# The local band of the first 288 tokens as dense blocks on TensorE, ahead of two MLPs

## Chip, cores and metric

One core of a Trainium2 chip runs the program. The metric is the device time of one execution in microseconds (us), the median over several runs. The engines are TensorE (PE; PEld is its weight load), VectorE (DVE), ScalarE (ACT), GpSimd (POOL) and SyncE (SP), which issues most DMAs.

## What is computed

For 4 batches, 8 heads, 576 tokens and 64 dimensions, each head adds two attentions. The coarse one works on means of four tokens (144 by 144); its result is repeated four times. The local one lets each query see the keys at a distance under four, a band of seven. The sum is a matrix of 2304 tokens by 512, which goes through two MLPs of width 2048.

```python
q_d = q.reshape(B, H, Sd, factor, D).mean(axis=3)      # k_d, v_d likewise, factor = 4
out_up = np.repeat(sm_attn(q_d, k_d, v_d), factor, axis=2)
mask = np.abs(pos[:, None] - pos[None, :]) < factor
scores = np.where(mask, scale * np.matmul(q, k.transpose(0, 1, 3, 2)), -1e9)
out = out_up + softmax(scores) @ v
r = np.maximum(x @ w_in, 0.0);  y = (s * (r * r) + b) @ w_out
h = y @ w_in2;  result = (h - np.tanh(h)) @ w_out2
```

## The kernel before

A batch is cut into two subs of 288 tokens, eight in all (s = 0 to 7). In the first MLP one sub is one tile of 288 columns (j = 0 to 7); the second MLP has six tiles of 384 columns. Every product runs as three products of split parts: a high part (`wah`, `wbh`, `xh`, `gh`) and a low part, the rest (`wal`, `wbl`, `xl`, `gl`).

**Band.** The partition holds a head pair and a chunk of 18 tokens. Sub 0 has the first nine tokens of every chunk, sub 1 the last nine, so each sub has tokens from all over the sequence. VectorE multiplies queries by seven shifted keys and sums over 64 dimensions (`key_products`, `key_sums`, in four units of 5, 5, 4 and 4 tokens), forms the softmax (`band_max`, `band_norm`, with the exponential on ScalarE) and multiplies and adds the values (`value_products`, `value_sums`). TensorE transposes the result (`columns`), and VectorE adds the coarse part `up` and writes `xraw` (`add_up`).

**Coarse attention.** POOL and VectorE add up groups of four tokens (`group_sums`), TensorE transposes them, and for each of eight steps (four head pairs, two halves of 72 queries) come `scores`, `score_max` (VectorE, tile `cneg`), `score_exp`, `score_inverse`, `score_scale`, `turn_probs` (a transpose), `place_probs`; `weigh` and `place_up` follow once per head pair.

**First MLP.** A turn is one of 16 slices f of the width: `hidden1` (12 products), then ScalarE's `activate1` (relu, `gh`, square), POOL's `g_low` (`gl`), then `output1` (12 products), three turns behind. Tile 0 needs each weight slice in two parts. ScalarE makes the high one (`w1_high`, L968). The low one is made for f under 8 (`FTURN`) by TensorE, as identity times raw minus high (`w1_rest`), and by ScalarE, which places it (`w1_place`); for the others by POOL (`w1_low`). Weights come in quarters of four slices, 1 MB each: `wa_raw` of `w_in`, `wb_raw` of `w_out`.

**Order.** Each engine runs its own list strictly in order. A planner (`Plan`) writes the lists out ahead of time from estimated costs and ranks. PE's small results go through two PSUM banks in turn (`pa`). A wait at the head of a list holds up all behind it. `add_up` of sub s waits until `hidden1` of tile s - 2 is done (`XRING`).

## Time and profile before

| | |
|---|---|
| median of 3 runs | 956.36 us (952.87 to 957.5) |
| the profiled execution | 955.23 us, its span 953.4 us |
| TensorE busy | 900.6 us, 94% |
| VectorE, ScalarE, POOL busy | 547.5, 429.6, 301.5 us |
| mean granted TensorE clock | 0.978 of full speed |

The profile is of one execution. Times count from the span's start. A row of a timeline has its start, its length, engine, line, operation, output<-input and count, and in square brackets how long the engine was idle before it and what ended that. A row by line has busy time, mean ns, and idle time before it. A row by stage reads, after the stretch and its length: busy us (and instruction count) of PE, PEld, VectorE, ScalarE and POOL, then the granted clock of TensorE as a share of 2.4 GHz, the busy share of the 16 DMA engines, and GB/s. Rows overlap on an engine by a few hundredths of a microsecond. A matmul in plain fp32 shows as two records.

### The profile page before, as it was taken

Reading aid. Unit: us, or ns where it says so; the run is one execution under the profiler, and the core shown is the slowest. Engines: PE = TensorE matmul, PEld = TensorE weight load, DVE = VectorE, ACT = ScalarE, POOL = GpSimd, SP = SyncE. Lnnn points to the kernel's source line nnn. Section 1 sums busy time; section 2 is a strip of 40 time slices with the busy share of each in tenths; the row PEclk is TensorE's granted clock in tenths of the full one; section 3 lists DMA queues with packets and bytes.
Section 4 is the critical chain, followed back from the end, with each engine's and each line's share of the span. In section 5 each row is a group of like instructions: output and inputs, shape, how many; then the busy total and the mean of one; then the engine's idle time right before and its main releaser. Section 6 shows DMA issues by size and latency. Waiting matters only on the chain.

```text
span 953.4 us, 14703 instructions
## 1 busy us (share of the span) xinstructions
PE 900.6 (94%) x5600; PEld 830.6 (87%) x5600; DVE 547.5 (57%) x630; ACT 429.6 (45%) x1081; POOL 301.5 (32%) x285
## 2 busy tenths in 40 slices
PE   1789879998999999999999999999999999999997
PEld 0348869998999899999999999999999999999996
DVE  6889999999998999983100462332332423322321
ACT  1688446455765477544645662322322323222221
POOL 6308975588747973344222200000000000000000
PEclk9779989999999999999999999999999999999999
DMA  9996024243424222201204430110100200100101
GB/s 226 260 240 145 25 72 132 59 123 99 111 61 124 62 71 67 68 1 34 92 1 148 153 103 1 34 34 1 55 12 1 67 1 1 34 1 1 34 1 33
DMA packets 35973, 66.47 MB, mean 70 GB/s; under 512 B 3920, under 2 KB 16192, under 8 KB 35904
## 3 DMA queue, kind: packets, MB, share of 16 engines
q1 hardware_dynamic: 33968, 62.39, 24.4%
q10 hardware_dynamic: 1936, 3.15, 1.5%
q8 instruction: 44, 0.72, 0.3%
q14 instruction: 25, 0.20, 0.1%
HBM read 56.09 MB, written 9.44 MB: 69 GB/s over the span
## 4 chain that ended last, share of the span: by engine, by line
PE 80%; DVE 9%; ACT 3%; issue 2%; DMA 2%; SPq 1%; POOL 1%; DVEq 0%; ACTq 0%
PE hid L1275 21%; PE acc L1293 21%; PE hid L1234 17%; PE acc L1256 17%; DVE prod L860 3%; DMA wa_raw<-in_moe_w_in_dram 2%; DVE prod L868 2%; DVE prod L873 1%; PE pa L1177 1%; PE pa L1202 1%; PE acc L1166 1%; DVE oloc L878 1%; PE pa L1188 1%; PE pa L1214 1%; SPq L618 1%
## 5 line engine op out<-in xcount | busy, mean ns | idle before, releaser
L740 POOL TENSOR_TENSOR gl<-relu,gh 128x288 fp32r<-128x288 f32 x128 | 146.3, 1144 | 193.8 <-PE acc L1256 160.0
L928 DVE TENSOR_TENSOR gdif<-hid,tanh 128x384 f32<-128x384 f32 x96 | 53.5, 557 | 184.8 <-ACT tanh L1115 184.8
L1234 PE MATMUL hid<-xh,wah 128*128 128x288 f32 x512 | 156.1, 306 | 0.0
L1256 PE MATMUL acc<-gh,wbh 128*128 128x288 f32 (+1 forms) x512 | 156.0, 305 | 0.0
L1234 PE MATMUL hid<-xh,wal 128*128 128x288 f32 x512 | 152.3, 299 | 0.0
L1256 PE MATMUL acc<-gl,wbh 128*128 128x288 f32 (+1 forms) x512 | 151.9, 297 | 0.0
L1256 PE MATMUL acc<-gh,wbl 128*128 128x288 f32 (+1 forms) x512 | 151.7, 296 | 0.0
L1234 PE MATMUL hid<-xl,wah 128*128 128x288 f32 x512 | 149.0, 298 | 1.8 <-POOL xl L731 1.8
L1115 ACT ACTIVATE tanh<-hid 128x384 f32<-128x384 f32 x96 | 47.1, 490 | 187.4 <-PE hid L1275 187.1
L1275 PE MATMUL hid<-x2h,wal 128*128 128x384 f32 x384 | 129.1, 336 | 0.0
L1275 PE MATMUL hid<-x2h,wah 128*128 128x384 f32 x384 | 129.0, 336 | 0.0
L1275 PE MATMUL hid<-x2l,wah 128*128 128x384 f32 x384 | 129.0, 336 | 0.0
L1074 ACT ACTIVATE relu<-hid 128x288 f32<-128x288 f32 x128 | 52.4, 409 | 148.5 <-PE hid L1234 141.2
L1293 PE MATMUL acc<-wbl,g2h 128*128 128x512 f32 x288 | 112.6, 391 | 0.0
L1293 PE MATMUL acc<-wbh,g2l 128*128 128x512 f32 x288 | 112.5, 391 | 0.0
L1293 PE MATMUL acc<-wbh,g2h 128*128 128x512 f32 x288 | 112.3, 390 | 0.0
L1256 PEld LDWEIGHTS acc<-gh,wbh 128*128 128x128 f32 x512 | 97.4, 190 | 2.4 <-issue 1.4
L1234 PEld LDWEIGHTS hid<-xh,wah 128*128 128x128 f32 x512 | 98.0, 191 | 1.6 <-issue 0.7
L1234 PEld LDWEIGHTS hid<-xl,wah 128*128 128x128 f32 x512 | 96.7, 191 | 2.3 <-POOL xl L731 2.3
L1234 PEld LDWEIGHTS hid<-xh,wal 128*128 128x128 f32 x512 | 98.0, 191 | 0.7
L1256 PEld LDWEIGHTS acc<-gh,wbl 128*128 128x128 f32 x512 | 97.1, 190 | 0.6
L1256 PEld LDWEIGHTS acc<-gl,wbh 128*128 128x128 f32 x512 | 96.9, 189 | 0.0
...
## 6 DMA issues: line engine op xcount, KB each, us to landing
...
ql<-in_q_dram SPq DMA_DIRECT2D x28, 144.0 KB, 3.2
```

The source lines that it names most:

```text
L618: sp.dma_start(stage_of(b, n).rearrange("p (h x) -> p h x", h=2), dram(v, b * BSTEP + 2 * hq * HSTEP + kh * HG * GROUP * HD, [[GROUP * HD, ...
L740: g.tensor_tensor(out=gl[:, turn % LRING1, 0:NS], in0=relu[:, f % 2, :], in1=gh[:, turn % GRING1, 0:NS].bitcast(F32), op=ALU.subtract).the ...
L860: ve.tensor_tensor(prod[:, 0:nt, :, :], vv, pv, ALU.mult).then_inc(s_mul, 1)
L868: ve.tensor_tensor(prod[:, 0:nt, 0:3, :], prod[:, 0:nt, 0:3, :], prod[:, 0:nt, 3:6, :], ALU.add).then_inc(s_tree, 1)
L873: ve.tensor_tensor(pairs, pairs, others, ALU.add).then_inc(s_tree, 1)
L928: ve.tensor_tensor(gdif[:, f % 2, :], hid[:, f % 2, 0:N2], tanh[:, f % 2, :], ALU.subtract).then_inc(s_dif, 1)
L1074: sc.activation(r, hid[:, f % 2, 0:n], ACT.Relu).then_inc(s_relu, 1)
L1115: sc.activation(tanh[:, f % 2, :], hid[:, f % 2, 0:N2], ACT.Tanh).then_inc(s_tanh, 1)
L1234: one = pe.matmul(dst, w[:, d, cols], x[:, j % XRING, d, :], start=i == 0, stop=i == len(products) - 1)
L1256: one = pe.matmul(acc[:, d, n], w[:, f, cols], g[:, turn % ring, n], start=(f == 0 and p == 0), stop=(f == FT - 1 and p == 2))
L1275: one = pe.matmul(hid[:, f % 2, 0:N2], w[:, d, f * P:(f + 1) * P], x[:, j % 2, d, :], start=(d == 0 and p == 0), stop=(d == KT - 1 and p = ...
L1293: one = pe.matmul(acc[:, i, :], g[:, f % GRING2, i * P:(i + 1) * P], w[:, f, :], start=(f == 0 and p == 0), stop=(f == FT - 1 and p == 2))
```

## The change

The tokens of batch 0 are split otherwise: sub 0 has tokens 0 to 287 in their own order, sub 1 the other 288, nine to a partition. Sub 0's band is no longer made on VectorE. For each head pair a (four):

- `dense_turn`: TensorE transposes keys and queries (three transposes each); VectorE copies the keys (`dense_keys`), ScalarE the queries (`dense_queries`), the two heads in separate columns.
- `dense_scores`: five products, each 60 queries of both heads by 66 keys.
- `dense_max`, `dense_exp`, `dense_norm`: mask, softmax over 66 columns, on VectorE, with the exponential on ScalarE.
- `dense_probs`, `dense_place`: five transposes, and ScalarE's copy.
- `dense_values`: ten products; `dense_add`: VectorE adds `up` and writes `xraw`. After it `xh` of this head pair may be made.

Keys, queries and values of sub 0 are loaded by token instead of by chunk, 64 floats at a time. The coarse attention of batch 0 does its first 72 queries for all four head pairs, then, behind the dense path, the other 72, with eight `weigh` steps of half the width. Tiles of the dense path lie where later weights go, so `wb_raw` of the last two quarters and `wbh` from f = 4 on wait for it. Low parts are now made by POOL in 24 of 32 cases and by TensorE in 8 (`low_maker`), and through `pa`. The add-up of sub 1 takes 15 instructions instead of 5. Stores of batch 0's rows follow the new order.

```diff
+BLOCKS, BSTEP1, BQ = 5, 57, 60
+BK = BQ + 2 * HALO
+BKEY0 = [0] + [BSTEP1 * i - HALO for i in range(1, BLOCKS)]
+DTOK = NS // 3
+DKEY = NS + HALO
...
+def low_maker(f, half):
+    return ("POOL", "POOL", "POOL", "PE")[(f + half) % 4]
...
+def score_of(b, i):
+    return (i % NPAIR, i // NPAIR) if b == 0 else (i // 2, i % 2)
+def weighs(b):
+    return 2 * NPAIR if b == 0 else NPAIR
...
+            if half and f >= WGROUP:
+                after.append(("dense_values", NPAIR - 1))
+            o.add("ACT", act(512), (2, f + 3 * half) if f + 3 * half > 3 else (1, 0, 5), ("w1_high", f, half), after)
+            maker = low_maker(f, half)
+            if maker == "PE":
+                o.add("PE", 1.1, (0, 9, f), ("w1_rest", f, half), [("w1_high", f, half)], 0.5, fills=True)
+                o.add("ACT", act(512), (0, 9, f), ("w1_low", f, half), [("w1_rest", f, half)],
+                      empties=("w1_rest", f, half))
...
+        o.add("DVE", 0.5, (0, 0, 30 + 0), ("dense_keys", a), [("dense_turn", a)] + ring)
...
+        o.add("PE", 2.4, (0, 0, 30 + 3), ("dense_values", a), [("dense_place", a), ("load_dense_values",)]
+              + {1: [("dense_keys", 3)], 2: [("dense_queries", 3)], 3: [("dense_add", 0)]}.get(a, []))
+        o.add("DVE", 0.55, (0, 0, 0), ("dense_add", a), [("dense_values", a), ("place_up", 0, a)])
...
+            if b == 0 and qh:
+                after.append(("dense_add", NPAIR - 1))
...
+    def tokens_of(s):
+        return (NS, SUB) if s == 1 else (s % NSUB * SUB, CHUNK)
...
+            elif kind == "load_dense_keys":
+                for j in range(3):
+                    sp.dma_start(dkey[0:DTOK, j, :, :], dram(k, j * HD, [[3 * HD, DTOK], [HSTEP, HEADS], [1, HD]])
+                                 ).then_inc(s_dkey, 16)
+                sp.dma_start(dkey[DTOK:DTOK + 1, :, :, :], dram(k, NS * HD, [[HD, 3], [HSTEP, HEADS], [1, HD]])
+                             ).then_inc(s_dkey, 16)
+            elif kind == "load_dense_queries":
+                for j in range(3):
+                    sp.dma_start(dqry[0:DTOK, j, :, :], dram(q, j * HD, [[3 * HD, DTOK], [HSTEP, HEADS], [1, HD]])
+                                 ).then_inc(s_dqry, 16)
...
+            elif kind == "load_dense_values":
+                for i in range(BLOCKS):
+                    sp.dma_start(dval[0:BK, i, :, :], dram(v, BKEY0[i] * HD, [[HD, BK], [HSTEP, HEADS], [1, HD]])
+                                 ).then_inc(s_dval, 16)
...
+                ve.tensor_tensor(pr[:, 0, :], s[:, 0, :], dmask[:, 0, :], ALU.add).then_inc(s_dmax, 1)
+                ve.tensor_tensor(pr[:, 1:BLOCKS, :], s[:, 1:BLOCKS, :],
+                                 over(dmask[:, 1, :], [[0, BLOCKS - 1], [1, BK]]), ALU.add).then_inc(s_dmax, 1)
+                ve.wait_ge(s_dmax, 4 * a + 2)
+                ve.tensor_reduce(mx, pr, AX_X, ALU.max).then_inc(s_dmax, 1)
+                ve.wait_ge(s_dmax, 4 * a + 3)
+                ve.tensor_tensor(pr, pr, over(mx, [[1, BLOCKS], [0, BK]]), ALU.subtract).then_inc(s_dmax, 1)
...
+                ve.tensor_reduce(sm, dprob[:, a % 2, :, :], AX_X, ALU.add).then_inc(s_dnorm, 1)
+                ve.wait_ge(s_dnorm, 3 * a + 1)
+                ve.reciprocal(iv, sm).then_inc(s_dnorm, 1)
+                ve.wait_ge(s_dnorm, 3 * a + 2)
+                ve.tensor_tensor(pr, pr, over(iv, [[1, BLOCKS], [0, BK]]), ALU.mult).then_inc(s_dnorm, 1)
...
+                ve.tensor_tensor(four(xraw[:, 0, a, :]), four(dense_out(a)),
+                                 over(up[:, a, 0:HG], [[1, HG], [0, GROUP]]), ALU.add).then_inc(s_dadd, 1)
...
+                if s == 1:
...
+                    for i, (t, c, group, chunks, groups) in enumerate(parts):
...
+                        uv = over(up[:, 0:1, group:group + 1], [[GROUPS, NPAIR]] + groups)
+                        ve.tensor_tensor(xv, pv, uv, ALU.add).then_inc(
+                            s_free[r] if i == len(parts) - 1 else s_added, 1)
...
+                sc.wait_ge(s_dmax, 4 * a + 4)
+                pr = dprob[:, a % 2, :, 0:BK]
+                sc.activation(pr, pr, ACT.Exp).then_inc(s_dexp, 1)
...
+                sc.activation(dpT[0:BK, a % 2, 0:4, :], acc[0:BK, 2, :].rearrange("p (i n) -> p i n", n=P), ACT.Copy
+                              ).then_inc(s_dpT, 1)
...
+                for j in range(3):
+                    one = pe.transpose(hid[:, 0, j * (DTOK + 1):(j + 1) * (DTOK + 1)],
+                                       pair(dkey[0:DTOK + 1, j, 2 * a:2 * a + 2, :]), ident[0:DTOK + 1, 0:DTOK + 1])
...
+                for i in range(BLOCKS):
+                    one = pe.matmul(acc[:, a % 2, i * BK:(i + 1) * BK], dqT[:, a % 2, i, :],
+                                    dkT[:, a % 2, BKEY0[i]:BKEY0[i] + BK], start=True, stop=True)
...
+                for i in range(BLOCKS):
+                    dst = acc[0:BK, 2, i * P:(i + 1) * P] if i < 4 else acc[0:BK, a % 2, 3 * P:4 * P]
+                    one = pe.transpose(dst, dprob[:, a % 2, i, 0:BK], ident[:, :])
...
+                for i in range(BLOCKS):
+                    n = BSTEP1 if i < BLOCKS - 1 else BQ
+                    for h2 in range(2):
+                        one = pe.matmul(dense_out(a)[h2 * HD:(h2 + 1) * HD, i * BSTEP1:i * BSTEP1 + n],
+                                        dval[0:BK, i, 2 * a + h2, :], dpT[0:BK, a % 2, i, h2 * HD:h2 * HD + n],
+                                        start=True, stop=True)
```

What the planner makes of it is seen in the lists. First the DMA queue of SyncE from the program's start, before the change; `own`, `first` and `firstv` are the coarse attention's tokens.

```order
L546 DMA kl<-in_k_dram 32x768
L546 DMA kl<-in_k_dram 31x192
L546 DMA kl<-in_k_dram 32x960
L546 DMA kl<-in_k_dram 32x2x960 x3
L613 DMA own<-in_q_dram 128x768 x2
L613 DMA first<-in_q_dram 128x768
L613 DMA first<-in_k_dram 128x768 x3
L618 DMA firstv<-in_v_dram 72x2x256 x8
L646 DMA wa_raw<-in_moe_w_in_dram 128x4x512
L655 DMA wb_raw<-in_moe_w_out_dram 128x4x512
L646 DMA wa_raw<-in_moe_w_in_dram 128x4x512
L655 DMA wb_raw<-in_moe_w_out_dram 128x4x512
```

And with the change:

```order
L736 DMA dkey<-in_k_dram 96x8x64 x3
L738 DMA dkey<-in_k_dram 1x24x64
L743 DMA dqry<-in_q_dram 96x8x64 x3
L723 DMA own<-in_q_dram 128x768 x2
L723 DMA first<-in_q_dram 128x768
L723 DMA first<-in_k_dram 128x768 x3
L748 DMA dval<-in_v_dram 66x8x64 x5
L728 DMA firstv<-in_v_dram 72x2x256 x8
L776 DMA wa_raw<-in_moe_w_in_dram 128x4x512
L613 DMA ql<-in_q_dram 32x2x576 x4
L621 DMA kl<-in_k_dram 32x2x960 x4
L776 DMA wa_raw<-in_moe_w_in_dram 128x4x512
L788 DMA wb_raw<-in_moe_w_out_dram 128x4x512
```

Three key loads, one small one, three query loads and five value loads of the dense path now stand ahead. Sub 1's `ql` and `kl` stand ahead of the second quarter of `w_in` and of the first of `w_out`. The window loads of sub 0 are gone (its `ql` and `vl` were on ScalarE's queue).

Second, ScalarE's list just ahead of tile 0, before the change (L968 makes high parts, L974 places low ones, L1065 makes `xh`):

```order
L968 ACTIVATE wbh<-wb_raw 128x512
L974 ACTIVATE wal<-acc 128x4x128
L968 ACTIVATE wah<-wa_raw 128x4x128
L968 ACTIVATE wbh<-wb_raw 128x512
L968 ACTIVATE wah<-wa_raw 128x4x128
L974 ACTIVATE wbl<-acc 128x512
L968 ACTIVATE wbh<-wb_raw 128x512
L974 ACTIVATE wal<-acc 128x4x128
L968 ACTIVATE wah<-wa_raw 128x4x128
L1065 ACTIVATE xh<-xraw 128x288 x4
L974 ACTIVATE wbl<-acc 128x512
```

And with the change (L1207 makes high parts, L1214 places low ones, L1320 makes `xh`):

```order
L1320 ACTIVATE xh<-xraw 128x288 x2
L1207 ACTIVATE wbh<-wb_raw 128x512
L1207 ACTIVATE wah<-wa_raw 128x4x128
L1295 ACTIVATE up<-pa 128x72
L1207 ACTIVATE wbh<-wb_raw 128x512
L1207 ACTIVATE wah<-wa_raw 128x4x128
L1207 ACTIVATE wbh<-wb_raw 128x512
L1207 ACTIVATE wah<-wa_raw 128x4x128
L1207 ACTIVATE wbh<-wb_raw 128x512
L1207 ACTIVATE wah<-wa_raw 128x4x128
L1320 ACTIVATE xh<-xraw 128x288
L1214 ACTIVATE wbl<-pa 128x512
```

All four `xh` stood together behind the eighth slice of the weights. Now three stand ahead, and the last one stands behind eight high parts, of which the first reads `wb_raw`.

Third, VectorE's list where sub 1 is worked on, before the change, key units and group sums:

```order
L799 TENSOR_REDUCE sc_72<-prod 128x35
L790 TENSOR_TENSOR prod<-ql,kl 128x2240
L799 TENSOR_REDUCE sc_72<-prod 128x35
L790 TENSOR_TENSOR prod<-ql,kl 128x1792
L799 TENSOR_REDUCE sc_72<-prod 128x28
L790 TENSOR_TENSOR prod<-ql,kl 128x1792
L810 TENSOR_TENSOR own<-own 128x6x64
L813 TENSOR_TENSOR qs<-own 128x192
L810 TENSOR_TENSOR own<-own 128x6x64
L813 TENSOR_TENSOR ks<-own 128x192
L799 TENSOR_REDUCE sc_72<-prod 128x28
```

And with the change:

```order
L997 TENSOR_REDUCE sc_72<-prod 128x35
L988 TENSOR_TENSOR prod<-ql,kl 128x2240
L948 TENSOR_TENSOR xraw<-acc,up 128x288
L997 TENSOR_REDUCE sc_72<-prod 128x35
L988 TENSOR_TENSOR prod<-ql,kl 128x1792
L966 TENSOR_REDUCE cneg<-pa 72x2 x2
L997 TENSOR_REDUCE sc_72<-prod 128x28
L988 TENSOR_TENSOR prod<-ql,kl 128x1792
L975 RECIPROCAL cinv<-csum 72x2 x2
L966 TENSOR_REDUCE cneg<-pa 72x2 x2
L997 TENSOR_REDUCE sc_72<-prod 128x28
L1029 SCALAR_TENSOR_TENSOR sc_72<-sc_72,mask 128x126
```

Three of the four `xraw` writes of sub 0 stand between sub 1's first key units, and the maxima of coarse steps 4 to 7 (L966) among the last ones. On TensorE the scores for the first two of these stand behind hidden turn 0, for the other two behind hidden turn 3. Further on, all six group sums of batch 1 that VectorE makes stand behind `band_norm` of sub 1; before, two stood there.

## Rows read from the trace of the kernel before

**Rows 1.** Section 1 of the page: busy time of each engine.
```profile
PE 900.6 (94%) x5600; PEld 830.6 (87%) x5600; DVE 547.5 (57%) x630; ACT 429.6 (45%) x1081; POOL 301.5 (32%) x285
```

**Rows 2.** Busy time by stage, columns as in the section on the profile.
```profile
0.00:34.90 34.90, 9.48 (x30) 4.22 (x30) 25.12 (x27) 9.52 (x32) 21.77 (x34) 1.00 0.96 234
34.90:74.00 39.10, 34.80 (x126) 18.75 (x127) 32.87 (x46) 31.83 (x90) 6.28 (x9) 0.74 1.04 246
74.00:144.00 70.00, 58.53 (x397) 54.21 (x395) 68.00 (x53) 40.22 (x108) 59.78 (x47) 0.93 0.30 75
144.00:550.70 406.70, 401.14 (x3038) 391.81 (x3037) 292.42 (x275) 231.44 (x623) 213.69 (x199) 0.99 0.30 84
550.70:953.40 402.70, 396.66 (x2016) 361.61 (x2015) 129.09 (x233) 116.62 (x230) 0.00 (x0) 1.00 0.08 22
```

**Rows 3.** Timeline of TensorE: first product of tile 0 and of tile 1.
```profile
73.95 0.29 PE L1234 MATMUL hid<-xh,wah 128*128 128x288 f32 x1
...
143.95 0.86 PE L1234 MATMUL hid<-xh,wah 128*128 128x288 f32 x1
```

**Rows 4.** VectorE by stretch: us, busy (x count), PEclk, DMA share, GB/s.
```profile
10.30:61.10 50.80, 46.54 (x54) 0.88 1.06 256
95.90:144.00 48.10, 47.52 (x37) 0.89 0.17 44
```

**Rows 5.** Chain of waits: start us, us, what.
```profile
153.95 3.19 PE hid L1234 x24
```

**Rows 6.** Timeline of VectorE, sub 1: start us, us, engine, line, operation.
```profile
89.69 2.00 DVE L799 TENSOR_REDUCE sc<-prod 128x28 f32<-128x1792 f32 x1
...
95.89 3.41 DVE L860 TENSOR_TENSOR prod<-vl,prob 128x2240 f32<-128x2240 f32 x1
99.22 1.64 DVE L810 TENSOR_TENSOR own<-own 128x384 f32<-128x384 f32 x1
100.90 0.85 DVE L813 TENSOR_TENSOR ks<-own 128x192 f32<-128x192 f32 x1
...
137.85 1.67 DVE L903 TENSOR_TENSOR xraw<-pa,up 128x256 f32<-128x256 f32 x3
```

**Rows 7.** VectorE by line, 10 to 61.2 us: busy us, mean ns.
```profile
L860 DVE TENSOR_TENSOR prod<-vl,prob 128x2240 f32<-128x2240 f32 x2 | 5.0, 2484 | 0.1
...
L878 DVE TENSOR_TENSOR oloc<-prod 128x320 f32<-128x320 f32 x2 | 1.0, 491 | 0.1
```

**Rows 8.** Timeline of ScalarE ahead of tile 0.
```profile
34.86 0.63 ACT L968 ACTIVATE wah<-wa_raw 128x512 fp32r<-128x512 f32 x1 [1.84 <-DMA wa_raw<-in_moe_w_in_dram]
...
67.39 0.62 ACT L968 ACTIVATE wbh<-wb_raw 128x512 fp32r<-128x512 f32 x1
67.91 0.62 ACT L968 ACTIVATE wah<-wa_raw 128x512 fp32r<-128x512 f32 x1
...
71.78 1.43 ACT L1065 ACTIVATE xh<-xraw 128x288 fp32r<-128x288 f32 x4
```

**Rows 9.** DMA from 35 to 40 us: packets; queue, MB, share of 16 engines.
```profile
DMA packets 944, 1.93 MB, mean 386 GB/s; under 512 B 36, under 2 KB 36, under 8 KB 944
...
q1 hardware_dynamic: 944, 1.93, 105.7%
```

**Rows 10.** DMA from 102 to 105 us, the same columns.
```profile
DMA packets 156, 0.15 MB, mean 49 GB/s; under 512 B 12, under 2 KB 156, under 8 KB 156
...
q1 hardware_dynamic: 156, 0.15, 18.5%
```

**Rows 11.** POOL by line, 0 to 150 us.
```profile
L740 POOL TENSOR_TENSOR gl<-relu,gh 128x288 fp32r<-128x288 f32 x17 | 25.8, 1521 | 10.7 <-PE acc L1256 8.7 <-ACT relu L1080 2.0
L726 POOL TENSOR_TENSOR wal<-wa_raw,wah 128x512 fp32r<-128x512 f32 x8 | 13.4, 1673 | 31.5 <-ACT wah L968 31.5
```

**Rows 12.** Timeline of TensorE: two low parts made by products.
```profile
47.67 1.07 PE L1166 MATMUL acc<-wb_raw,ident 128*128 128x512 f32 x2
...
48.80 1.02 PE L1166 MATMUL acc<-wa_raw,ident 128*128 128x512 f32 x2
```

More of the change, by code:

```diff
@@ L244, in plan @@
-    for s in range(SUBS):
+                o.add("PE", 0.4, (0, b, 8 + 2 * i), ("weigh", b, w), after, lead(b), fills=True)
+                o.add("ACT", 0.22, (1, b, 9 + 2 * i), ("place_up", b, w), [("weigh", b, w)], empties=("weigh", b, w))
+    for s in range(1, SUBS):
         b = s // NSUB
-        for i, (kind, loads, kbytes) in enumerate((("load_queries", 4, 600), ("load_keys", 5, 1000),
-                                                   ("load_values", 5, 1000))):
+        for i, (kind, loads, kbytes) in enumerate((("load_queries", 4, 600), ("load_keys", 4, 1000),
+                                                   ("load_values", 4, 1000))):
@@ L579, in wait_sums, with dense_out @@
         e.wait_ge(s_vsums if vector_sums(b, n) else s_sums, sums_count(b, n))
+    low_of = {}
+    for engine in ("POOL", "DVE", "ACT"):
+        for n, step in enumerate(one for one in o.order[engine] if one[0] == "w1_low"):
+            low_of[step] = n + 1
     def wait_low(e, f, half):
-        if f < FTURN:
-            e.wait_ge(s_w1place, 2 * f + half + 1)
-        else:
-            e.wait_ge(s_w1low, 2 * (f - FTURN) + half + 1)
+        maker = low_maker(f, half)
+        count = low_of["w1_low", f, half]
+        if maker == "PE":
+            r, m = bank("w1_rest", f, half)
+            e.wait_ge(s_free[r], m)
+        else:
+            e.wait_ge(s_w1vlow if maker == "DVE" else s_w1low, count)
+    high_of = {step: n + 1 for n, step in enumerate(one for one in o.order["ACT"] if one[0] == "w1_high")}
+    def dense_out(a):
+        return (acc[:, 3, 0:NS], hid[:, 0, 0:NS], hid[:, 1, 0:NS], acc[:, 3, 0:NS])[a]
     def turned(raw):
@@ L1157, in tensor_program @@
                 f, half = key
-                if f == 0 and half == 0:
-                    pe.wait_ge(s_ident, 2)
-                    pe.wait_ge(s_minus, 1)
-                dst = acc[:, f % 2 * 2 + half, :]
-                if f > 1:
-                    pe.wait_ge(s_w1place, 2 * (f - 2) + half + 1)
-                pe.wait_ge(s_w1high, 2 * f + half + 1)
-                pe.matmul(dst, ident[:, :], half_of(f, half, wa_raw, wb_raw), start=True, stop=False)
-                pe.matmul(dst, minus[:, :], half_of(f, half, wah, wbh), start=False, stop=True).then_inc(s_w1rest, 1)
+                r = room(kind, *key)
```

461 lines of the change are left out of this document (318 added, 143 removed).

## Prediction

> **What bounds the kernel now.** I read the totals, then the busy time by stage. TensorE is busy for 94% of the span [rows 1], so most of the time is dense products and only what happens around them can move. The stages [rows 2] show where: from 144.0 to 550.7 us TensorE is busy 401 of 407 us, and after 550.7 us 397 of 403 us. The change does not touch those products. Two stretches are different. Until 74 us the big products have not begun: TensorE's first product of `hidden1(0,0)` starts at 73.95 [rows 3]. The DMA engines are full there (share 0.96 and 1.04 [rows 2]). From 74 to 144 us TensorE is busy 58.5 of 70 us at a mean granted clock of 0.93 of 2.4 GHz, while VectorE is busy 68.0 [rows 2], and from 95.9 us on 47.5 of 48.1 [rows 4]. Tile 0 of the first MLP holds 16 hidden turns and 13 output turns before tile 1 begins; 24 products take 3.19 us [rows 5], so 0.133 each and 1.60 per turn: 46.3 us of work fill 70 us. Tile 1 starts at 143.95 [rows 3], 4.4 us after VectorE's last add-up of sub 1 (137.85 + 1.67 = 139.5 [rows 6]). So two things decide the time: when tile 0 starts, and when VectorE has finished sub 1. What comes after 143.95 shifts with it as a block.
>
> Could tile 2 or later wait for VectorE instead? In 144.0 to 550.7 us VectorE is busy 292 of 407 us [rows 2], so it has room; I add no wait there.
>
> **The sum.** It is made against the profiled execution's own 955.2 us (span 953.4 plus 1.8); the median of the runs shown is 956.4, so 1.1 us are added at the end.
>
> *Removed and added on VectorE.* Sub 0's band is gone: VectorE was busy 46.5 us from 10.3 to 61.1 [rows 4], most of it this band. The dense path costs VectorE, per head pair, a copy, two mask adds, a maximum, a subtraction, a sum, a reciprocal, a scaling and an add, on 66 to 335 columns. Nearest row: 0.49 us for 320 elements [rows 7]; seven such and two short ones make 3.6 us, 14 us for four pairs. This lies in the time in which everything waits for loads, so I count it as hidden. Without that cover it would cost up to 14 us, still less than the 36 us or so that it replaces. Its 104 small TensorE products and its ScalarE copies lie there too.
>
> *Loads before the first weights.* Today the first quarter of `w_in` is usable at 34.86 us: ScalarE's first `wah` ends its idle time on that DMA [rows 8]. Sub 0's `ql`, `kl` and `vl` go from the front of the queues: 2.55 MB, at 234 GB/s [rows 2] 10.9 us. In their place come keys, queries and values with one run of 64 floats per token and head: 3 x 96 x 8 + 24, 3 x 96 x 8 and 5 x 66 x 8, together 7,272 packets of 256 bytes. No row has that size. Nearest: from 35 to 40 us 908 data packets of 2,125 bytes on average took 105.7% of 16 engines for 5 us, 93 ns each [rows 9]; from 102 to 105 us 144 packets of 1,024 bytes took 18.5% for 3 us, 61 ns each [rows 10]. The line through both gives 39 ns at 256 bytes. Lower end: in proportion to bytes, 11 ns. Upper end: no cheaper than 1,024 bytes, 61 ns. I take 39, since the two rows show a fixed part of about 31 ns. That is 7,272 x 39 / 16 = 17.7 us (5.1 to 27.7). The first weights land at 34.9 - 10.9 + 17.7 = 41.7 us.
>
> The Trainium skill's page "DMA: Bandwidth & Descriptors" says two things here. Its section "Specifications" wants at least 512 bytes for line rate and says that smaller transfers are read, modified and written; that speaks against this change. Its section "Why small descriptors are slow (HBM only)" puts the loss of a 256-byte descriptor at 3 cycles on 8, which would put the packets near 15 ns, an estimate with which the sum would be about 11 us lower. The trace has a fixed part far above 3 in 8; it shows no packet of this size.
>
> *To the first turn.* ScalarE's order has `xh` for the last head pair behind eight weight halves, and the first `wbh` of them needs the first quarter of `w_out`. Ahead of that quarter now stand sub 1's `ql` and `kl` and a second quarter of `w_in`: 3.67 MB with itself, at 246 GB/s [rows 2] 14.9 us, so it lands at 56.6. Then eight halves at 0.52 (67.91 - 67.39) and one `xh` at 0.36 (1.43 / 4) [rows 8]: 61.3 with `up`. On POOL the last `xl` stands behind three low parts of 1.67 and costs up to 1.52, the price of a `gl` [rows 11]: 57.1 + 5.0 + 1.5 = 63.6. The first hidden turn ends at about 63.8. Today it begins at 73.95.
>
> *VectorE's sub 1.* Its key products begin when `kl` has landed, some 7 us behind 41.7, and run until the maxima of coarse scores 6 and 7. TensorE issues those behind hidden turn 3: 63.8 + 0.8 for scores 4 and 5, + 3 x 1.60, + 0.8 = 70.2, and 0.9 for the two maxima is 71.1. Before, from the start of the last key sum to the first value product it took 95.89 - 89.69 = 6.2 us [rows 6]. So value products begin at 77.3 instead of 95.9. Today the rest takes 139.5 - 95.9 = 43.6 us. Changes in it: six group sums instead of two, (1.64 + 0.85) [rows 6] each, +10.0; one key product less, -2.5 (a product of that size is 2.48 [rows 7]); three maxima and two reciprocals less, -1.6; fifteen add-ups instead of five, ten short ones more at 0.23, +2.3. That is 51.8, and 4.4 more to the first product: tile 1 starts at 133.5 us, 10.5 earlier.
>
> I keep today's slow durations (value product 3.41 [rows 6] against 2.48 undisturbed [rows 7]): POOL works in the same stretch today, 59.8 of 70 us [rows 2], and the change gives it 24 low parts instead of 16.
>
> *Is another engine later?* TensorE from 63.8: 28 turns 44.8; six low parts made by products of identity and raw weights, 48.80 - 47.67 = 1.13 each [rows 12], 6.8; 67 small products, between 0.13 [rows 5] and 0.38 (a third of 1.13), taken at 0.19, 12.6: it would be ready at 128.0. POOL from 57: 24 x 1.6 + 16 x 1.5 [rows 11] + eight `xl` at 1.1 = 71: 128. Both are within 6 us of VectorE's 133.5, so VectorE decides, but narrowly.
>
> *After tile 1's start.* Two more score products and eight more transposes of batch 0 or 1 fall into tile 1: ten at 0.13 [rows 5], -1.3 us of the gain. Output rows in the new token order make a few more stores in stage two, beside 397 us of products [rows 2]: nothing; if the last store grew it would cost under 3 us, but only early tiles change.
>
> Sum: 955.2 - 10.5 + 1.3 = 946.0, and with 1.1 the forecast is **947 us**.
>
> **Rivals.**
>
> *B, more is gained.* The packets go nearer to their bytes (20 ns: 8.6 us earlier, at 0.4545 us per ns) and VectorE is disturbed less, so that TensorE's own path decides: 128.0 - 8.6 = 119.4, a gain of 24.5 - 1.3 us, 933 us. For it: some 30 us of VectorE work vanish and the undisturbed rows are much shorter. Against it: POOL's load rises, and in-order engines that are all nearly full have lost time here.
>
> *C, no change.* A 256-byte packet costs what one of 1,024 bytes does, 61 ns: 10.0 us later everywhere, 957 us. The transfers eat the band's gain. It holds from 49 ns up to 70.
>
> *D, slower.* Each short run is moved in two passes, a read and a write back, 2 x 39 = 78 ns: 17.7 us more, 965 us. The place is the start of the load queue, ahead of every weight. It decides from 70 ns on (946.9 + 31 x 0.4545 = 961). The rows on packets neither show nor exclude it, since the shortest one that they price has 1,024 bytes. This is the rule of the section "Specifications" of the Trainium skill's page "DMA: Bandwidth & Descriptors".
>
> That the change does not do what it says: if ScalarE's in-order wait for the first `w_out` quarter came much later, tile 0 would start as today although VectorE is free. That is C by another way and is in its chance.
>
> **Chances and range.** Forecast (942 to 952) 0.47, B (926 to 941) 0.26, C (952 to 961) 0.15, D (above 961) 0.12. A measurement of this kernel can tell about 0.5%, 4.8 us: faster is below 951.6. Nearly all of the forecast's case and all of B are faster, 0.71; C and the forecast's edge are the same, 0.17; slower 0.12. The range reaches from inside B to the end of C: 932 to 960; the forecast's own is 942 to 952.
>
> **What would show it.** Short packets: the DMA share and packets of the first 15 us give the price; right is 30 to 49 ns. First `wah` on ScalarE at 39 to 45 us with its idle time ended by the DMA; first `wbh` 13 to 17 us later, also by the DMA. First hidden turn ends near 64. VectorE's first value product of sub 1 near 77, its wait before by coarse scores 6 and 7. Last add-up of sub 1 near 129, first product of tile 1 near 133, and from there 408 us to the end of the first MLP. The prediction is wrong if the first `wah` comes after 50 us, if TensorE rather than VectorE sets tile 1's start, or if tile 2 or a later tile waits for VectorE.

## The result and the profile after

The changed kernel took 941.32 us (median of 4 runs, 940.53 to 943.46), the kernel before 955.15 beside it: ratio 0.986, interval 0.983 to 0.989. It is faster by 1.4%, 13.8 us. The forecast was 947 us. The profiled execution took 940.56 us, where the sum had 946.0.

The totals after (the answer to [rows 1]):

```profile
PE 897.9 (96%) x5763; PEld 836.5 (89%) x5763; DVE 522.8 (56%) x641; ACT 432.0 (46%) x1096; POOL 319.3 (34%) x298
```

Busy time by stage, cut at the first product of tile 0, the first of tile 1 and the end of the first MLP, with the columns of [rows 2]:

```profile
0.00:34.90 34.90, 22.54 (x151) 17.51 (x152) 19.68 (x51) 17.90 (x56) 23.07 (x43) 1.00 0.91 231
34.90:50.70 15.80, 11.03 (x96) 7.84 (x97) 13.56 (x12) 10.71 (x29) 10.54 (x7) 0.57 1.05 265
50.70:125.60 74.90, 66.58 (x459) 59.58 (x458) 69.19 (x73) 51.80 (x144) 61.81 (x44) 0.95 0.46 128
125.60:534.60 409.00, 400.78 (x3049) 389.99 (x3048) 289.87 (x273) 234.30 (x639) 223.90 (x206) 1.00 0.31 85
534.60:938.50 403.90, 396.97 (x2017) 361.55 (x2015) 130.47 (x235) 117.27 (x232) 0.00 (x0) 1.00 0.08 22
```

Tile 0 starts 23.3 us earlier (73.95 in [rows 3]) and takes 74.9 us instead of 70.0, so tile 1 starts 18.4 us earlier. From there to the end of the first MLP it is 409.0 us instead of 406.7 [rows 2], and behind it 403.9 instead of 402.7: 18.4 - 2.3 - 1.2 = 14.9 us of span.

TensorE's timeline: first product of tile 0, of its hidden turn 4, the wait for VectorE's results, the first transposes of batch 1, coarse scores of batch 1 that waited for a buffer emptied by VectorE's last add-ups, and the first product of tile 1:

```profile
50.70 0.29 PE L1549 MATMUL hid<-xh,wah 128*128 128x288 f32 x1
...
61.88 0.40 PE L1549 MATMUL hid<-xh,wah 128*128 128x288 f32 x1 [1.09 <-POOL wal L873]
...
89.31 0.87 PE L1529 MATMUL pa<-ident,oloc 128*128 128x128 f32 x3 [3.70 <-DVE oloc L1076]
...
98.16 0.82 PE L1408 MATMUL pa<-ident,qs 128*64 128x128 f32 x6
...
115.57 1.16 PE L1488 MATMUL pa<-kT,qT 128*72 128x288 f32 x4 [1.18 <-DVE xraw L1107]
...
125.59 0.30 PE L1549 MATMUL hid<-xh,wah 128*128 128x288 f32 x1
```

VectorE's timeline: last add of the dense path, first value product of sub 1, two later ones, the first add-up, a key product of sub 2, and the last add-ups:

```profile
47.76 0.45 DVE L948 TENSOR_TENSOR xraw<-acc,up 128x288 f32<-128x288 f32 x1
...
67.82 2.49 DVE L1058 TENSOR_TENSOR prod<-vl,prob 128x2240 f32<-128x2240 f32 x1
...
80.62 3.56 DVE L1058 TENSOR_TENSOR prod<-vl,prob 128x2240 f32<-128x2240 f32 x1
...
91.87 2.02 DVE L1058 TENSOR_TENSOR prod<-vl,prob 128x1792 f32<-128x1792 f32 x1
...
96.48 0.99 DVE L1107 TENSOR_TENSOR xraw<-pa,up 128x128 f32<-128x128 f32 x5
...
107.20 1.39 DVE L1076 TENSOR_TENSOR oloc<-prod 128x256 f32<-128x256 f32 x1
...
114.10 1.87 DVE L1107 TENSOR_TENSOR xraw<-pa,up 128x64 f32<-128x64 f32 x10
```

VectorE is through with sub 1 at 116.0, 9.6 us before tile 1 begins, against 4.4 before. The chain of work that ended last runs through VectorE from 66.8 us to the wait at 115.57, and from there to tile 1 it is TensorE's own queue: five turns and the coarse scores between them, 10.0 us without a wait.

ScalarE's first high parts (the answer to [rows 8]): the first `wah` has no idle time ahead of it now, the first `wbh` waited for its load:

```profile
31.80 0.61 ACT L1207 ACTIVATE wah<-wa_raw 128x512 fp32r<-128x512 f32 x1
...
43.51 0.63 ACT L1207 ACTIVATE wbh<-wb_raw 128x512 fp32r<-128x512 f32 x1 [1.16 <-DMA wb_raw<-in_moe_w_out_dram]
```

The DMA view from 5 to 8 us, when nearly all packets are the short ones of the dense blocks. 118.9% of 16 engines for 3 us over 2,685 packets is 21.3 ns each; the share is above 100%, so packets overlap on an engine, and the 48 engine-microseconds over as many packets give 17.9 ns:

```profile
DMA packets 2689, 0.70 MB, mean 233 GB/s; under 512 B 2680, under 2 KB 2680, under 8 KB 2689
...
q1 hardware_dynamic: 2685, 0.70, 118.9%
```

Last, GpSimd's timeline around 80 us. It is to be read against VectorE's row at 80.62. VectorE's value product took 3.56 us instead of 2.49 and ended at 84.18; GpSimd's subtraction took 3.54 and ended at 85.34, 1.16 us behind it. The rows fit two engines that take turns and don't run beside each other: VectorE waited 1.22 us until the subtraction before had ended (81.84) and then needed 2.34, GpSimd waited 2.38 us and then needed 1.16.

```profile
80.45 1.39 POOL L873 TENSOR_TENSOR wal<-wa_raw,wah 128x512 fp32r<-128x512 f32 x1
81.80 3.54 POOL L873 TENSOR_TENSOR wbl<-wb_raw,wbh 128x512 fp32r<-128x512 f32 x1
```

For comparison, a subtraction beside a reduction of VectorE, where neither is longer than elsewhere:

```profile
59.59 2.00 DVE L997 TENSOR_REDUCE sc<-prod 128x28 f32<-128x1792 f32 x1
```

```profile
60.55 1.27 POOL L873 TENSOR_TENSOR wal<-wa_raw,wah 128x512 fp32r<-128x512 f32 x1
```

The Trainium skill's page "SBUF — State Buffer" says so in its section "Who interferes with whom": an operation of VectorE with both inputs in SBUF and one of GpSimd that reads SBUF share a pair of ports, and the second waits until the first is done; a reduction doesn't contend. Both pairs of rows agree: 3.56 and 3.54 us in the first, 2.00 and 1.27 us in the second.

### The profile page after: what moved, and what is told of

It is laid out like the page before. It is cut to its first block, busy times and chain, and to the rows that moved or that the text cites. A ratio compares the mean times of both kernels' runs of the same rounds, so it can differ in the third digit from the quotient of the medians.

```text
span 938.5 us, 15072 instructions
## 1 busy us (share of the span) xinstructions
PE 897.9 (96%) x5763; PEld 836.5 (89%) x5763; DVE 522.8 (56%) x641; ACT 432.0 (46%) x1096; POOL 319.3 (34%) x298
## 4 chain that ended last, share of the span: by engine, by line
PE 76%; DVE 12%; issue 3%; ACT 3%; DMA 3%; SPq 2%; DVEq 0%; ACTq 0%
PE acc L1606 21%; PE hid L1588 21%; PE hid L1549 16%; PE acc L1569 15%; DVE prod L1058 3%; DMA wb_raw<-in_moe_w_out_dram 3%; DVE prod L1066 2%; DVE prod L1071 2%; DVE oloc L1076 1%; PE pa L1488 1%; DVE sc L997 1%; ACT pc L1250 1%; PE pa L1516 1%; SPq L748 1%; DVE own L1008 1%
## 5 line engine op out<-in xcount | busy, mean ns | idle before, releaser
L887 POOL TENSOR_TENSOR gl<-relu,gh 128x288 fp32r<-128x288 f32 x128 | 133.0, 1041 | 179.1 <-PE acc L1569 141.4
L1143 DVE TENSOR_TENSOR gdif<-hid,tanh 128x384 f32<-128x384 f32 x96 | 53.5, 557 | 182.8 <-ACT tanh L1370 182.8
L1549 PE MATMUL hid<-xh,wal 128*128 128x288 f32 x512 | 150.4, 295 | 0.0
L1549 PE MATMUL hid<-xl,wah 128*128 128x288 f32 x512 | 146.8, 294 | 0.0
L1588 PE MATMUL hid<-x2h,wah 128*128 128x384 f32 x384 | 129.0, 336 | 0.8 <-DVE gdif L1143 0.8
L1588 PE MATMUL hid<-x2h,wal 128*128 128x384 f32 x384 | 129.0, 336 | 0.0
## 6 DMA issues: line engine op xcount, KB each, us to landing
wb_raw<-in_moe_w_out_dram SPq DMA_DIRECT2D x8, 1024.0 KB, 11.4
```

The costliest lines, as they stand in the source:

```text
L887: g.tensor_tensor(out=gl[:, turn % LRING1, 0:NS], in0=relu[:, f % 2, :], in1=gh[:, turn % GRING1, 0:NS].bitcast(F32), op=ALU.subtract).the ...
L1143: ve.tensor_tensor(gdif[:, f % 2, :], hid[:, f % 2, 0:N2], tanh[:, f % 2, :], ALU.subtract).then_inc(s_dif, 1)
L1549: one = pe.matmul(dst, w[:, d, cols], x[:, j % XRING, d, :], start=i == 0, stop=i == len(products) - 1)
L1588: one = pe.matmul(hid[:, f % 2, 0:N2], w[:, d, f * P:(f + 1) * P], x[:, j % 2, d, :], start=(d == 0 and p == 0), stop=(d == KT - 1 and p = ...
```

## The experiments

Four theories were told apart, A to D with a few variants: **A**, TensorE's own queue (its work and the waits that stand in it) fills tile 0; **B**, VectorE's last add-up decides, as predicted; **C** or P, GpSimd's low parts pace it; **D**, VectorE and GpSimd take turns, and what both have to do fills it. V is B in a wider form: all that VectorE has to do on the way paces tile 0. Most edits are moves in the planned queues: `(engine, steps, behind which step)`. Each ratio is to the kernel before as measured beside that run (medians of 954.7 to 956.9 us), while differences to the changed kernel are between medians of different sessions and are good to about 2 us.

**1. Twice the short packets.** Behind each dense load:

```
+ sp.dma_start(<memory not used yet>, dram(k, j * HD, [[3 * HD, DTOK], [HSTEP, HEADS], [1, HD]])).then_inc(s_twice, 16)
+ # the same for the queries and values; load_w1a 2 waits for s_twice
```

> The changed kernel, and behind each load of the dense blocks the same load once more into memory that is not used yet: 7,248 packets of 256 bytes more ahead of the first weights. By the price that the trace of the changed kernel shows (19 to 20 ns) that is 8.8 us of 16 engines; by the prediction's 39 ns it would be 17.7. If the load queue decides when tile 0 starts, hidden turn 4 starts at 70 to 71 instead of 61.9 and the time is 949 to 951 us. If ScalarE's and VectorE's work decides it, 941 to 944. With the prediction's price, 958 and more.

951.45 us, ratio 0.995 (0.993 to 0.997): 10.1 us more than the changed kernel, just above the range for the load queue. Its first turn started at 61.32 and its hidden turn 4 at 73.50, 11.6 later:

```profile
61.32 0.29 PE L1559 MATMUL hid<-xh,wah 128*128 128x288 f32 x1
...
73.50 0.40 PE L1559 MATMUL hid<-xh,wah 128*128 128x288 f32 x1 [1.09 <-POOL wal L883]
```

So what stands ahead of the weights in the load queue reaches the end whole, and 10.1 x 16 / 7,248 = 22 ns is a packet's price, near the row above. By the ratios the difference is 8.1 us (18 ns), and the first `wbh` comes 10.9 us later (54.4 instead of 43.5, 24 ns), so the price is known as 18 to 24 ns, not closer.

**2. The first turn earlier.**

```
+ ("ACT", [w1_high 1 0], place_up 0 0), ("ACT", [w1_high 2 0], place_up 0 2), ("ACT", [x_high 0 3], place_up 0 3)
+ ("DVE", [dense_add 3], key_sums 1 0), ("POOL", [w1_low 1 0], w1_low 0 0), ("POOL", [w1_low 2 0], x_low 0 2)
+ ("POOL", [x_low 0 3], w1_low 0 1), ("PE", [w1_rest 2 1, w1_rest 3 0], hidden1 0 0)
+ # the first hidden turn waits for the last dense add-up
```

> The changed kernel with the queues around the first hidden turn in another order: ScalarE splits the high halves of hidden turns 1 and 2 before the first quarter of w_out is there, and the last xh ahead of four halves; GpSimd makes the low parts of hidden turns 1 and 2 in time in which it waited; VectorE's last dense add-up stands ahead of the second key product; TensorE's first hidden turn ahead of its two products for low parts. It should start at 46.5 to 47.5 instead of 50.7. Theory A (tile 1 follows TensorE's queue): the start is given on whole, 3 to 4 us, 937 us. Theory B (VectorE sets tile 1): its key part waits for coarse scores 6 and 7 behind hidden turn 3, which also come earlier, but it has its products to do: 1 us or less. Theory C (GpSimd paces tile 0): two low parts are out of its queue, 3.5 us or more, 936.

944.72 us, 0.989 (0.986 to 0.992): a miss for all three. The first product came at 45.63, 5.1 us earlier, but the turn's last one waited for GpSimd until 50.10, and the two pairs of products for low parts, which had filled the wait ahead of the turn, now stood behind it at half the granted clock (1.2 GHz until 53.5). Turn 4 started at 64.2, 2.3 later than in the changed kernel.

```profile
45.63 0.58 PE L1571 MATMUL hid<-xh,wah 128*128 128x288 f32 x1 [2.10 <-issue]
...
50.10 0.61 PE L1571 MATMUL hid<-xl,wah 128*128 128x288 f32 x1 [1.48 <-POOL xl L898]
50.50 1.91 PE L1436 MATMUL pa<-wb_raw,ident 128*128 128x512 f32 x2
```

**3. The waits out of TensorE's queue.**

```
+ ("PE", [columns 1 0, w1_rest 14 1], hidden1 0 9), ("PE", [columns 1 1, columns 1 2], hidden1 0 12)
+ ("PE", [scores 1 0, scores 1 1], output1 0 10)
```

> The changed kernel with one thing else: in TensorE's queue of tile 0 the transposes of sub 1's results stand later (the first group behind hidden turn 9, two turns later; the other two behind hidden turn 12, one turn later; the first two coarse scores of batch 1 behind output turn 10). Theory A (TensorE's own queue sets the start of tile 1: turns, small products and its waits for VectorE in the queue): the wait of 3.70 us at 89.31 goes, with it the 6.8 us at half the clock behind it (worth 3.4), and some 2 of the 2.15 us at 108.74 and 115.57: 6 to 9 us earlier, 932 to 936 us. Theory B (VectorE's last add-up sets it): nothing is earlier, 940 to 943, since the add-ups come later if anything. Theory C (GpSimd's low parts pace tile 0): the wait moves to a low part, 938 to 941.

946.46 us, 0.990 (0.987 to 0.993): slower than the changed kernel by 5 (by 4 going by the ratios), a miss for all three. The wait of 3.70 fell to 0.53, and another of 9.51 came:

```profile
103.50 1.49 PE L1423 MATMUL pa<-ident,qs 128*64 128x128 f32 x6 [9.51 <-DVE xraw L1122]
```

The buffer that these transposes fill is emptied by VectorE's first add-up, which stands behind its third value sum. In the changed kernel that add-up ran at 96.48, because VectorE had run undisturbed from 91 on while GpSimd waited 4.90 us for TensorE (the value product at 91.87 took 2.02). Here GpSimd went on, and the same value product took 3.08:

```profile
95.41 3.08 DVE L1073 TENSOR_TENSOR prod<-vl,prob 128x1792 f32<-128x1792 f32 x1
```

With the moves of 2 added:

> The moves of columns_later and of first_turn_earlier together. Theory A: the gains add up, 928 to 932 us. Theory C (GpSimd paces tile 0): little more than the larger one of the two, 935 to 937.

948.34 us, 0.992 (0.989 to 0.995), the same 9.51 us wait at 105.62, and a miss for both theories: gains that were none add up to none.

**4. The add-up earlier too.** As 3, and `("DVE", [add_up 1 0], group_sums 1 3)`.

> As columns_later, and VectorE's first add-up of sub 1 stands right behind the fourth group sum of batch 1 instead of behind the third value sum, so that the buffer that TensorE's transposes waited 9.51 us for at 103.50 comes free at about 96. Theory A (TensorE's queue): that wait shrinks to 1 or 2 us and the saving of the waits shows at last, 934 to 937 us. Theory D (VectorE's operations with two inputs in SBUF and GpSimd's take turns, and what both have to do fills tile 0 from hidden turn 4 on; a wait taken out of TensorE's queue lets GpSimd work where VectorE ran undisturbed before): from hidden turn 4 to tile 1 it stays 63 to 65 us, as in the changed kernel (63.7) and in first_turn_earlier (64.8), and the time is 940 to 944.

941.27 us, 0.984 (0.981 to 0.987), no different from the changed kernel, and 63.7 us from turn 4 (62.55) to tile 1 (126.27), as D had it. The 9.51 us became 2.46 at 95.70, and the next wait for VectorE came up, for a group sum:

```profile
105.28 0.61 PE L1424 MATMUL pa<-ident,ks 128*64 128x128 f32 x2 [4.11 <-DVE ks L1027]
```

**5. More work for VectorE**, behind the last value sum, on top of 3; first two reductions, then two operations with two inputs:

```
+ ve.tensor_reduce(sc0[:, 0:5, :], prod[:, 0:5, :, :], AX_X, ALU.add)                          # vector_more, twice
+ ve.tensor_tensor(prod[:, 0:5, :, :], prod[:, 0:5, :, :], prod[:, 0:5, :, :], ALU.max)        # pair_more, twice
```

> As columns_later, and VectorE does two more reductions of 2,240 elements (2.48 us each, nothing uses them) behind the last value sum of sub 1, 5 us ahead of the last add-ups. Theory A (TensorE's queue): within 1.5 us of columns_later, since VectorE was through 9.6 us before tile 1 began. Theory B (VectorE's last add-up): 5 us more than columns_later.

> As vector_more, but the two added operations of VectorE have two inputs in SBUF (maximum of the products with themselves, 2,240 elements) instead of one. Undisturbed a product of that size takes 2.48 us, the same as the reduction. Theory A and any theory by which only VectorE's own time or only its last add-up counts: as vector_more, 946 to 948. Theory D (taking turns): the 5 us of added work hold GpSimd's low parts up too, and TensorE waits for those: 3 to 6 us more than vector_more, 949.5 to 953.

946.48 us (0.990, 0.987 to 0.993) and 946.25 (0.989, 0.987 to 0.991) against 946.46. Theory B is out in its strict form: 5 us more of VectorE ahead of its last add-ups cost nothing. The add-ups themselves came later by less than 5 us, for in experiment 3 they had waited 2.86 us for TensorE. These are their rows in `columns_later`, `vector_more` and `pair_more`:

```profile
117.36 1.92 DVE L1122 TENSOR_TENSOR xraw<-pa,up 128x64 f32<-128x64 f32 x10 [2.86 <-PE pa L1544]
```

```profile
120.87 1.90 DVE L1129 TENSOR_TENSOR xraw<-pa,up 128x64 f32<-128x64 f32 x10
```

```profile
120.90 1.88 DVE L1129 TENSOR_TENSOR xraw<-pa,up 128x64 f32<-128x64 f32 x10
```

Counted from the first value product they are 2.1 and 3.5 us later, and from their end to tile 1 it is 8.7 and 8.5 us instead of 11.3. D missed as well: the two operations took 5.51 us, 0.5 more than undisturbed, and GpSimd, which had caught up and then stood idle for 8.73 us, had only two operations to do beside them. That the two engines take turns should cost only where both are full; this case fits that and does not prove it.

```profile
109.38 5.51 DVE L1098 TENSOR_TENSOR prod<-prod 128x2240 f32<-128x2240 f32 x2
```

**6. Less work for GpSimd, with and without more for TensorE.** First, the products use the high part again in place of those low parts:

```
+ if f >= 8: raw, hi, lo = (t[:, 0:1, 0:2] if half == 0 else t[:, 0:2] for t in (raw, hi, lo))
```

> The changed kernel without the low parts of both weights for hidden turns 8 to 15, as far as GpSimd makes them: GpSimd's twelve subtractions shrink to two elements a row, and TensorE multiplies by the high part once more in their place, so its work is the same. Theory D (VectorE's operations with two inputs in SBUF and GpSimd's take turns): VectorE does the same operations from the first value product to the last value sum of sub 1 in about 25 to 30 us instead of 40.8, its first value products of 2,240 elements stay slow but those from 80 us on take 2.0 to 2.5 instead of 3.1 to 3.6; from hidden turn 4 to tile 1 it takes 55 to 59 us instead of 63.7: 933 to 937 us. If VectorE's durations don't hang on GpSimd, they stay and the time is 940 to 943.

932.34 us, 0.975 (0.974 to 0.977): 9.0 us less than the changed kernel, slightly better than D's 933 to 937. VectorE's value products of the second and the fourth unit of sub 1, which took 3.56 and 3.10 us in the changed kernel:

```profile
78.54 2.49 DVE L1060 TENSOR_TENSOR prod<-vl,prob 128x2240 f32<-128x2240 f32 x1
...
94.43 2.01 DVE L1060 TENSOR_TENSOR prod<-vl,prob 128x1792 f32<-128x1792 f32 x1
```

The same operations took 30.8 us from the first value product to the last value sum (68.29 to 99.10) instead of 40.8. By stretch from turn 4 to tile 1, first this kernel, then the changed one:

```profile
62.30:117.40 55.10, 53.67 (x390) 48.67 (x391) 50.31 (x64) 43.53 (x119) 34.12 (x37) 1.00 0.40 104
```

```profile
61.90:125.60 63.70, 56.47 (x390) 50.41 (x391) 58.94 (x63) 43.42 (x119) 52.35 (x37) 0.95 0.35 89
```

TensorE's 390 instructions now take 53.67 us of 55.10: here its own work fills the stretch. In the changed kernel the stretch is 8.6 us longer. Of that 2.8 us are products at a lower clock (56.47 - 53.67; the granted clock was 0.69 from 89.3 to 98.2, behind the wait of 3.70 us), and 5.9 us are waits for VectorE (total us, times, longest):

```profile
PE pa L1529 <- DVE oloc L1076: 4.7, 2, 3.7
PE pa L1488 <- DVE xraw L1107: 1.2, 1, 1.2
```

`lows_out` has neither of them. The waits for ScalarE are 1.3 us in both stretches. TensorE waits for a low part of GpSimd only once, at turn 4, 1.1 us in both kernels. So GpSimd's low parts don't pace tile 0 directly (C); they lengthen VectorE's operations, and for those TensorE waits.

Then the half of the low parts instead of a quarter by TensorE and ScalarE, `low_maker` being `("POOL", "PE")[(f + half) % 2]`:

> The changed kernel with half of the low parts of the weights made by TensorE and ScalarE instead of a quarter: eight less on GpSimd (1.27 us each undisturbed, 10 us, and the turns that they take from VectorE), eight more pairs of products on TensorE (1.13 each, 9 us) and copies on ScalarE (0.6 each). The planner orders the queues anew. Theory A (TensorE's queue is what fills tile 0): 5 to 9 us later, 946 to 950. Theory D (VectorE and GpSimd together fill it): 10 us of the shared time go and TensorE fills the waits that it has (9 us from 52 on): 935 to 940.

949.75 us, 0.993 (0.990 to 0.995), slower by 8.4. TensorE's busy time from turn 4 to tile 1 rose from 56.47 to 66.47 us, the stretch from 63.7 to 74.1:

```profile
62.10:136.20 74.10, 66.47 (x429) 56.62 (x427) 65.19 (x76) 54.20 (x151) 52.99 (x44) 0.93 0.42 111
```

This is A's number, and a miss for D. The planner's new order is in it too, and 39 more instructions lie in the stretch, so it doesn't show that the products alone cost it.

**7. Less work for VectorE.** Without four group sums of batch 1, and with all six moved behind sub 1:

```
+ if b == 1 and n > 1: pairs, rest, dst, even, odd = (t[:, 0:1, 0:2] for t in (pairs, rest, dst, even, odd))   # sums_out
+ rank of group_sums: (0, b, n) if b == 0 else (1, b, 10 + n)                                                  # sums_last
+ ("DVE", [add_up 1 0], value_products 1 2), ("DVE", [add_up 1 1, add_up 1 2], group_sums 1 1),
+ ("PE", [columns 1 1, columns 1 2], hidden1 0 12)
```

> The changed kernel with four of the six group sums of batch 1 (the last of its queries and its keys) left out but for two elements: coarse attention of batch 1 is computed from other sums. They took 6.5 us of VectorE (two inputs in SBUF; 3.6 undisturbed) between 91.0 and 101.0. Theory D (taking turns): 3.5 to 6.5 us earlier, 935 to 938. Theory A (TensorE's queue): only the later waits of 0.97 and 1.18 us go, 939 to 940.

> The changed kernel with VectorE's six group sums of batch 1 behind all value sums of sub 1 instead of between them, its first add-up directly behind the third value product, the other two add-ups ahead of the first key product of sub 2, TensorE's transposes of batch 1 behind hidden turn 13, and those of sub 1's results where their data come. Nothing is left out. Theory V (what VectorE has to do up to the last add-up paces tile 0, through the waits that stand in TensorE's queue): 10 us of VectorE's work move behind tile 1's start, so hidden turn 4 to tile 1 takes 54 to 59 us instead of 63.7, and if tile 2 doesn't wait for VectorE the time is 932 to 937 us; each microsecond that tile 2 waits is lost again. Theory A (TensorE's own work fills tile 0, its waits are made up anyway): 939 to 942.

`sums_out`: 938.73 us, 0.981 (0.979 to 0.983); from turn 4 to tile 1 60.0 us instead of 63.7. Its first turn came 2.5 us later than in the changed kernel's profile, which hides as much. The time lies between D's range and A's; the 3.7 us in the stretch are within D's 3.5 to 6.5.

`sums_last`: 956.27 us, 1.001 (0.999 to 1.002), a clear miss. Tile 1 did start earlier, at 123.7, and would have by up to 6 us more without a wait for the moved sums. But tile 2 started at 198.2 instead of 187.8: from the end of tile 1's last hidden turn (187.7) TensorE was busy 4.8 of 10.5 us. VectorE's work was moved, not removed, and sub 2 came later. The longest wait there was for GpSimd's third group sum of queries, which ended at 195.6 instead of 176.5; why GpSimd was that late was not taken apart.

```profile
114.57 0.82 PE L1423 MATMUL pa<-ident,qs 128*64 128x128 f32 x3 [5.97 <-DVE qs L1026]
...
195.72 0.60 PE L1423 MATMUL pa<-ident,qs 128*64 128x128 f32 x2 [4.30 <-POOL qs L882]
```

**8. VectorE's part of sub 1 earlier.**

```
+ ("SP", [load_queries 1, load_keys 1], load_stage 0 13), ("SP", [load_w1b 0], load_w1a 0)
+ ("DVE", [key_products 1 0], ends), ("DVE", [key_sums 1 0], dense_add 0), ("DVE", [key_products 1 1], dense_add 2)
+ ("DVE", [key_sums 1 3], score_inverse 0 5), ("DVE", [band_norm 1], band_max 1), ("ACT", [band_exp 1], score_scale 0 5)
+ # and eleven moves around the first turn, much as in 2; ("PE", [w1_rest 14 1], hidden1 0 8)
```

> A version that starts VectorE's part of sub 1 earlier, with nothing left out: the queries and keys of sub 1 are loaded ahead of the first quarter of w_in and the first quarter of w_out ahead of the second of w_in; VectorE's first key product lies in its wait at 34.80 to 37.01 and its last key sum ahead of the maxima of coarse scores 6 and 7; ScalarE makes the band's exponentials two steps earlier; the first turn's order is as in first_turn_earlier, but with TensorE's two products for low parts ahead of it; one product for a low part stands ahead of TensorE's wait at 89.31. Theory V (VectorE's work in a row, from its first key product to the last add-up of sub 1, paces tile 0, slowed by GpSimd): value products start at 62 to 64 instead of 67.8 and tile 1 4 to 6 us earlier, 935 to 938 us. Theory P (GpSimd's low parts pace it, VectorE has room): tile 1 follows the first turn or the low parts, 1 us or less, 940 to 942. If both hold each other up, the value products start at 62 to 64 but take longer than 40.8 us up to the last value sum, and 938 to 940 is left.

941.66 us, 0.986 (0.984 to 0.988), no different: a miss for V, and the number of P. The value products started at 64.52, 3.3 us earlier, and the last value sum ended at 105.26, 3.3 earlier: the same 40.7 us. Tile 1 still started at 125.9, since the first add-up (98.26) was 1.8 us later than in the changed kernel and TensorE waited for it; from 61.9 us to 125.6 TensorE waited 6.6 us for VectorE and 2.0 for a low part, so P's number is met without P's wait:

```profile
64.52 2.49 DVE L1090 TENSOR_TENSOR prod<-vl,prob 128x2240 f32<-128x2240 f32 x1
...
98.26 0.97 DVE L1139 TENSOR_TENSOR xraw<-pa,up 128x128 f32<-128x128 f32 x5
```

```profile
99.29 0.42 PE L1440 MATMUL pa<-ident,qs 128*64 128x128 f32 x1 [6.58 <-DVE xraw L1139]
```

**What they show together.** In eight kernels tile 1 starts a nearly fixed time after the first transposes of batch 1 that can only follow VectorE's first add-up, because they need its buffer:

| kernel | those transposes | tile 1 | between |
|---|---|---|---|
| changed kernel | 98.16 | 125.6 | 27.4 |
| columns_later | 103.50 | 130.6 | 27.1 |
| vector_more | 104.95 | 131.5 | 26.6 |
| pair_more | 103.56 | 131.3 | 27.7 |
| first_turn_earlier | 100.79 | 129.0 | 28.2 |
| both_moves | 105.62 | 132.3 | 26.7 |
| packets_twice | 110.11 | 138.4 | 28.3 |
| vector_ahead | 99.29 | 125.9 | 26.6 |

Where work or waits behind the transposes change, so does the time: 25.0 us in `lows_out` (92.4 to 117.4) and `sums_out` (99.8 to 124.8), and 30.6 in `columns_and_add_up` (95.7 to 126.3), where the wait of 4.11 us lies behind them. The stretch behind the transposes, first the changed kernel, then `lows_out`:

```profile
98.20:125.60 27.40, 25.26 (x181) 23.47 (x180) 27.03 (x29) 16.41 (x49) 24.81 (x19) 1.00 0.22 53
```

```profile
92.40:117.40 25.00, 25.00 (x181) 23.62 (x180) 24.56 (x31) 16.56 (x49) 15.77 (x19) 1.00 0.23 58
```

So tile 0 has two parts. Up to there VectorE sets the pace, slowed by GpSimd: in the changed kernel through the wait of 3.70 us and the lower clock behind it, in five others through a wait of 6.6 to 9.5 us at the transposes themselves. Behind them TensorE's own queue is 25 us long, and VectorE's later results add about 2 us of waits. No theory met all its numbers. D had `columns_and_add_up`, nearly `lows_out`, and missed `pair_more` and `lows_on_pe`; A had `vector_more`, `pair_more` and `lows_on_pe` and missed `columns_later` and `both_moves`.

## Why the prediction came out right, and where its steps were off

The mechanism was right as far as the earlier start of tile 0 and VectorE's pace go. That the number came as near as it did is partly luck: of tile 1's start, value products 9.5 us earlier and the rest of sub 1 3.6 us shorter than forecast were offset by a tail 5.2 us longer.

**Short packets: mis-sized.** Taken at 39 ns, bounds 11 and 61; measured 18 to 24, so at 21.3 ns 9.7 us for all of them instead of 17.7. The fixed part of 31 ns, read off a line through two rows of long packets, isn't there at 256 bytes. The Trainium skill's page "DMA: Bandwidth & Descriptors" says in its section "Specifications" that transfers under 512 bytes are read, modified and written; the 78 ns of rival D are not there, but 21 ns is about twice the price in proportion to bytes (11 ns), so no run here rules a second pass out. The 3 cycles on 8 of the page's section "Why small descriptors are slow (HBM only)", an estimate of 15 ns, were nearer than the line.

**To the first turn: right in direction, wrong in what ends it.** First weights landed not at 41.7 but at 29.8 (issued at 20.5, 9.3 us to landing); ScalarE came to them only at 31.80, so they decided nothing. First quarter of `w_out` at 43.5 instead of 56.6. Of these 13.1 us the packets explain 8.0 at 21.3 ns, the rate of 265 GB/s instead of 246 another 1.1. The other 4 lie ahead of the first weights (11.9 us early, 8.0 by the packets): either the loads taken out were worth more than the 10.9 us set for them, or the packets cost less than 21.3 ns, which no run separates. First hidden turn ends at 52.4 instead of 63.8.

**VectorE's sub 1.** Value products at 67.8 (forecast 77.3), from there to the last add-up 48.2 us (51.8). The maxima of coarse scores 6 and 7 (58.73) had no wait ahead of them: VectorE was busy with its own key products until 57.9, so these scores delayed nothing that the profile shows. ScalarE's order added a wait of 1.79 us for the exponentials. To keep today's slow durations was right: less disturbed, the value part took 10 us less (experiment 6).

**"VectorE decides, but narrowly": the step that failed.** VectorE is the chain up to 115.4 us, as forecast; what failed is that tile 1 follows its last add-up by a fixed 4.4 us. Last add-up at 116.0 (129.1), then 9.6 us to tile 1, because TensorE's queue behind its wait for these add-ups holds 10.0 us of its own work. With the add-ups 2 to 3.5 us later and 5 us more for VectorE nothing changed (5). The prediction's own sign, that TensorE rather than VectorE sets tile 1's start, is met for this last part. From the end of the first hidden turn to tile 1 it took 73.2 us (125.6 - 52.4), where 69.7 were forecast (133.5 - 63.8), so 3.5 of the 11.4 us that this turn ended early were lost. Tile 1 at 125.6 instead of 133.5, 7.9 earlier.

**After tile 1's start.** 409.0 us against 408, and 1.2 us in stage two for which nothing was set. With the 0.2 us more that lie outside the span this makes the sum: 946.0 - 7.9 + 1.0 + 1.2 + 0.2 = 940.5, against 940.56 measured.

**The rivals.** B's condition held (packets near 20 ns), but not its second half: GpSimd, with 24 low parts, disturbed VectorE as before (value products of 3.56 and 3.10 us). `lows_out`, with twelve of these low parts gone, came to 932, near B's 933. The prediction's rivals C and D are out by the packets' price.

Not shown: no run undid the token order, the halves of the coarse queries or the planner's new costs one by one, so their shares of the 13.8 us aren't known; the 2.3 us more in tiles 1 to 7 weren't taken apart. No version without work left out beat the changed kernel.
